# A second layer by seven quarter products, in two phases, in a fused attention and two-layer kernel

## The reference

```python
# q, k, v: 2 x 8 heads x 768 x 64; window 128 and 4 sink keys
a = softmax(where(is_sink | in_window, q @ k.T / 8, -1e9)); x = (a @ v)      # 1536 tokens x 512
h = x @ w_in                                  # layer one, 512 -> 1024
solu = h * softmax(h); ln = (solu - mean) / sqrt(var + 1e-6) * g_ln
x2 = ln @ w_out                               # 1024 -> 512
h2 = x2 @ w2_in                               # layer two, 512 -> 2048
return (maximum(h2, 0) ** 2) @ w2_out         # 2048 -> 512
```

## Time and profile before

| | us |
|---|---|
| timed runs: median (lowest to highest, 3 runs) | 484.2 (483.32 to 484.57) |
| the profiled execution: span | 481.6 |
| TensorE busy | 471.1 |
| VectorE, ScalarE, GpSimd busy | 278.1, 212.9, 103.8 |

### The profile page before, as it was taken

The page is one execution under the profiler, slowest core; times in us unless marked ns, Lnnn a source line. Parts: engine busy times, 40 slices in busy tenths (PEclk is TensorE's granted clock), DMA queues, the critical chain, the costliest instruction groups (busy, mean ns, idle before and its releaser), DMA issues.

```text
span 481.6 us, 7337 instructions
## 1 busy us (share of the span) xinstructions
PE 471.1 (98%) x2634; PEld 382.5 (79%) x2634; DVE 278.1 (58%) x514; ACT 212.9 (44%) x559; POOL 103.8 (22%) x155
## 2 busy tenths in 40 slices
PE   7889999999999999999999999999999999999997
PEld 5667787887788888878888888888888888888885
DVE  3899889898989888767755354322222233222232
ACT  3677777656777666242324253222222232222221
POOL 2366323231321232739930000000000000000000
PEclk9999999999999999999999999999999999999999
DMA  7931437765569424498400000200000020000002
GB/s 214 315 92 50 136 85 215 205 192 159 149 180 219 113 57 120 119 252 240 90 1 0 1 0 1 87 0 0 0 0 0 0 87 1 0 0 1 0 1 87
DMA packets 51990, 41.80 MB, mean 87 GB/s; under 512 B 28088, under 2 KB 38072, under 8 KB 51448
## 3 DMA queue, kind: packets, MB, share of 16 engines
q1 hardware_dynamic: 51192, 40.74, 29.9%
q10 hardware_dynamic: 768, 0.66, 0.5%
HBM read 30.38 MB, written 11.01 MB: 86 GB/s over the span
## 4 chain that ended last, share of the span: by engine, by line
PE 91%; DVE 3%; POOL 2%; ACT 1%; DMA 1%; issue 1%; ACTq 0%; DVEq 0%; POOLq 0%
PE score_ps L1675 27%; PE h_ps L1689 14%; PE w_ps L1516 13%; PE h_ps L1476 12%; PE w_ps L1689 7%; PE wt_ps L1689 7%; PE o_ps L1438 4%; PE score_ps L1404 2%; PE wt_ps L1404 2%; PE wt_ps L1415 1%; DMA x2T<-qT 1%; PE o_ps L1459 1%; POOL pT_own L576 1%; PE w_ps L1541 1%; DVE prob L1095 1%
## 5 line engine op out<-in xcount | busy, mean ns | idle before, releaser
L1675 PE MATMUL score_ps<-x2T_hi,w2in_hi 128*128 (+1 forms) x192 | 74.8, 389 | 0.0
L1675 PE MATMUL score_ps<-x2T_hi,w2in_lo 128*128 (+1 forms) x192 | 74.7, 389 | 0.0
L1675 PE MATMUL score_ps<-x2T_lo,w2in_hi 128*128 (+1 forms) x192 | 74.7, 389 | 0.0
L1328 DVE TENSOR_TENSOR e<-e 128x512 f32<-128x512 f32 x24 | 17.9, 744 | 82.0 <-ACT e L968 82.0
L1328 DVE TENSOR_TENSOR sq<-relu 128x512 f32<-128x512 f32 x24 | 17.2, 717 | 77.0 <-ACT relu L968 77.0
L968 ACT ACTIVATE relu<-score_ps 128x512 f32<-128x512 f32 x24 | 14.3, 597 | 90.5 <-PE score_ps L1675 90.5
L968 ACT ACTIVATE e<-score_ps 128x512 f32<-128x512 f32 x24 | 14.4, 599 | 89.7 <-PE score_ps L1675 89.7
L1675 PEld LDWEIGHTS score_ps<-x2T_lo,w2in_hi 128*128 128x128 f32 x192 | 36.0, 188 | 7.5
L1675 PEld LDWEIGHTS score_ps<-x2T_hi,w2in_hi 128*128 128x128 f32 x192 | 36.1, 188 | 7.5
L1675 PEld LDWEIGHTS score_ps<-x2T_hi,w2in_lo 128*128 128x128 f32 x192 | 36.0, 188 | 7.4
L742 ACT ACTIVATE prob<-sm,nbias 128x132 f32<-128x132 f32 (+1 forms) x96 | 37.6, 393 | 4.1 <-DVE nbias L1019 3.4
(11 more groups left out here) (192 smaller groups left out, 1095.0 us busy)
## 6 DMA issues: line engine op xcount, KB each, us to landing
u_dram<-uT SPq DMA_DIRECT2D x18, 256.0 KB, 3.2
...
w2in<-w_in SPq DMA_DIRECT2D x4, 1024.0 KB, 5.3
...
V<-v SPq DMA_DIRECT2D x12, 256.0 KB, 3.2
x2T<-x_dram SPq DMA_DIRECT2D x12, 256.0 KB, 4.8
x_dram<-x SPq DMA_DIRECT2D x44, 64.0 KB, 2.2
...
```

Of the source, the lines that this page charges most:

```text
L1328: nc.vector.tensor_tensor(sq[f % 2], relu[f % 2], relu[f % 2], ALU.mult).then_inc(sq_ready, 1)
L1675: done = mm(h2_ps[f % 2], ws[:, c, fs], xs[:, c, bass.ts(blk, BLK)], start=(c == 0 and i == 0), stop=(c == MC - 1 and i == 2))
```

## The change

Layer two is done in two phases, and its activation g (16 chunks by all 1536 tokens) is kept whole in SBUF.

Phase one makes g. The tokens are two passes of 768, each in two halves of 384 columns; the hidden chunks are eight pairs j = (chunk j, chunk j + 8). For pairs 0 and 1 each of four quarters (one chunk, one half) is a plain product: 12 matmuls of 384 columns (`quarter`). For pairs 2 to 7 the 2 x 2 block product (two chunks by two halves, the contraction of 512 in two halves of 256) is computed from seven products of sums of quarters instead of eight (`multiply`: 2 passes x 2 contraction chunks x 3 matmuls, 384 columns each). The sums of weights are made by GpSimd per pair (`sum_w2`: four operations of 256 elements; `split_w2`: 512, 512, 512 and 256 elements), the sums of activations once per pass (`sum_x`, `split_x` on VectorE, `round_x` on ScalarE, 768 elements each), and the results are put together in g by ScalarE (copies `copy_p1`, `corner`) and VectorE (five additions of 768 elements, then `gate_row`: relu times itself on 1536). Weights of w2_in are loaded pair by pair.

Phase two multiplies g with w2_out, token tile by token tile: 48 matmuls of 512 columns per tile, g split per tile (`round_g`, `split_g`). w2_out is loaded in eight pieces of two chunks (`wy`) through two raw buffers; the first two tiles go in turns of 4, 4 and 8 chunks. The places of most of these tensors are those of tensors of before that are dead by then.

In layer one, project(9) is cut after 8 of its 24 matmuls, the rest stands behind hidden(11); project(10) writes another PSUM bank than project(11) and the transposes (`x2_bank`), so that `transpose_ln(11)` waits for one square_x2 less; last tile's squares have a place of their own. The loops (`Fori`) of block_b are gone: all is straight-line.

The core of the diff; the removed functions of layer two are those described above, and the small functions left out (`sum_x`, `split_x`, `round_x`, `sum_w2`, `split_w2`, the five additions, `copy_y`) wait for what they read and do one operation each, as told above:

```diff
 QUADS = P // SQ
 MOVES = 16 * QUADS
-NB = T // BLK
-TB = BLK // P
-X2T_AT = (7, 11)
+PASSES = 2
+TS = T // PASSES
+TH = TS // 2
+QH3 = TH // P
+NJ = C2 // 2
+CLASSIC = 2
+QUARTERS = ((0, 0), (1, 0), (1, 1), (0, 1))
+BLOCKS = tuple((j, s) for s in range(PASSES) for j in range(CLASSIC))
+A11, A12, S3, A22, S1, S2, S4 = range(7)
+B11, T2, B21, T3, T1, T4, B22, B12 = range(8)
+PRODUCTS = ((A11, B11, 0, True), (S2, T2, 1, True), (A12, B21, 0, False), (S3, T3, 1, False),
+            (S1, T1, 0, True), (A22, T4, 1, False), (S4, B22, 0, False))
+NP = len(PRODUCTS)
+P_FIRST, P_SECOND, P_CORNER, P_THIRD, P_LOWER, P_LEFT, P_RIGHT = range(NP)
+EARLY_TILES = 2
 LN_EPS, SM_EPS = 1e-6, 1e-9
 
...
+quarter_ps = [score_ps[:, 0:TH], score_ps[:, BANK:BANK + TH]]
+prod_pairs = [(score_pair, wt_pair), (h_pair, wo_pair)]
+y_ps = [score_ps[:, 0:BANK], score_ps[:, BANK:2 * BANK], w0_ps, tr_ps,
+        h_ps[:, 0:BANK], h_ps[:, BANK:2 * BANK], w1_ps, o_ps]
...
+    def load_w2(j):
+        if since(j, 2):
+            sp.wait_ge(w2_split, w2_parts_before(j - 1))
+        for r in range(2):
+            cols = slice((r * NJ + j) * P, (r * NJ + j + 1) * P)
+            sp.dma_start(w2_raw[j % 2][:, :, r, :], w2_in[:, cols].rearrange("(c p) f -> p c f", p=P)
+                         ).then_inc(w2_loaded[j % 2], 16)
+    def load_wy(j):
+        sp.wait_ge(*((wy_split, j - 1) if j >= 2 else (w2_split, w2_parts_before(NJ - 1 + j))))
+        sp.dma_start(wy_raw[j % 2][:, :, :],
+                     w2_out.rearrange("(r j p) m -> p r j m", r=2, p=P)[:, :, j, :]
+                     ).then_inc(wy_loaded[j % 2], 16)
...
+    load_x2T(1, TPB, TPB + QH3, x2T_loaded[1])
     store_x2(NT - 3)
-    load_x2T(1)
-    sp.wait_ge(h_done, 2 * NT)
-    for c in range(C2 // 2):
-        sp.dma_start(w2out[:, 2 * c:2 * c + 2, :],
-                     w2_out[2 * c * P:(2 * c + 2) * P, :].rearrange("(c p) m -> p c m", p=P)
-                     ).then_inc(w2out_loaded[c], 16)
+    sp.wait_ge(lnT_split, len(LN_PARTS) * (NT - 1))
+    load_w2(1)
+    load_w2(2)
     store_x2(NT - 2)
+    load_x2T(1, TPB + QH3, NT - 1, x2T_loaded[2])
     store_x2(NT - 1)
-    load_x2T(2)
-    with sp.Fori(0, NB - 1) as blk:
-        for i in range(TB):
-
-            sp.wait_ge((y_copied_act, y_copied_dve)[i % 2], TB // 2 * blk + (i // 2 + 1))
-            sp.dma_start(out[bass.ds(blk * BLK + i * P, P), :], y[i]).then_inc(y_stored, 16)
-    for i in range(TB):
-        cols = slice(0, DM // 2 if i == TB - 1 else DM)
-        sp.wait_ge((y_copied_act, y_copied_dve)[i % 2], TB // 2 * (NB - 1) + i // 2 + 1)
-        sp.dma_start(out[(NB - 1) * BLK + i * P:(NB - 1) * BLK + (i + 1) * P, cols], y[i][:, cols]
-                     ).then_inc(y_stored, 16)
-    sp.wait_ge(y_stored, 16 * (TB * NB + 1))
+    load_x2T(1, NT - 1, NT, x2T_end_loaded)
+    for j in range(3, NJ):
+        load_w2(j)
+    for j in range(NJ):
+        load_wy(j)
...
+    split_w2(0)
+    inverse_std(NT - 1)
+    split_w2(1)
+    for j in range(CLASSIC, NJ):
+        sum_w2(j)
+        split_w2(j)
...
+    def drain(n):
+        j, s = BLOCKS[n // len(QUARTERS)]
+        r, h = QUARTERS[n % len(QUARTERS)]
+        act.wait_ge(multiplied, n + 1)
+        nc.scalar.copy(g[:, j, r, s * TS + h * TH:s * TS + (h + 1) * TH], quarter_ps[n % 2]).then_inc(corner_ready, 1)
+    def copy_p1(j):
+        act.wait_ge(multiplied, multiplied_before(j) + P_FIRST + 1)
+        nc.scalar.copy(corner_of(j, 1, 0), pair_of(j, 0)).then_inc(p1_copied, 1)
+    def corner(j):
+        act.wait_ge(multiplied, multiplied_before(j) + P_CORNER + 1)
+        nc.scalar.copy(corner_of(j, 0, 0), pair_of(j, 0)).then_inc(corner_ready, 1)
+    def round_wy(j):
+        act.wait_ge(wy_loaded[j % 2], 16 * (j // 2 + 1))
+        act.wait_ge(multiplied, multiplied_before(NJ - 1) + (P_CORNER + 1, P_THIRD + 1, NP)[min(j, 2)])
+        nc.scalar.activation(wy[j][:, :, 0, :], wy_raw[j % 2][:, :, :], ACT.Copy).then_inc(wy_rounded, 1)
+    def round_g(t, part):
+        chunks = g_parts(t)[part]
+        act.wait_ge(g_ready, gates_before(NJ - 1 if len(g_parts(t)) > 1 and part == 0 else NJ))
+        if t < 2:
+            act.wait_ge(multiplied, multiplied_before(NJ - 1) + (P_CORNER + 1, P_LEFT + 1)[t])
+        else:
+            act.wait_ge(y_done, t - 1)
+        nc.scalar.activation(g_hi[t % 2][:, chunks, :], g_tile(t, chunks), ACT.Copy).then_inc(g_rounded, 1)
...
+    round_x(0, B11)
+    round_x(0, B21)
+    round_w2(0)
     hidden_exp(NT - 1)
     hidden_sum(NT - 1)
+    round_x(0, B12)
     for part in range(len(LN_PARTS)):
         round_lnT(NT - 2, part)
+    drain(0)
+    round_x(0, B22)
     for part in range(len(LN_PARTS)):
         round_lnT(NT - 1, part)
+    drain(1)
+    round_w2(1)
+    round_x(0, T1)
+    round_x(0, T2)
+    round_x(0, T3)
+    act.wait_ge(x2_done, NT)
+    round_x(1, B11)
+    round_x(1, B21)
+    for n in range(2, 7):
+        drain(n)
+    round_x(1, B12)
+    round_x(1, B22)
+    drain(7)
+    round_x(0, T4)
+    drain(8)
+    drain(9)
+    act.wait_ge(t_summed[0], 4)
+    round_x(1, T1)
+    round_x(1, T2)
+    drain(10)
+    round_x(1, T3)
+    drain(11)
+    round_w2(2)
+    for n in range(12, 16):
+        drain(n)
+    round_x(1, T4)
+    for j in range(CLASSIC, NJ):
+        copy_p1(j)
+        corner(j)
+        if j + 1 < NJ:
+            round_w2(j + 1)
+    round_g(0, 0)
+    round_wy(0)
+    round_wy(1)
+    round_g(1, 0)
+    round_wy(2)
+    round_wy(3)
+    round_g(0, 1)
+    round_g(1, 1)
+    for j in range(4, NJ):
+        round_wy(j)
...
+    def split_wy(j):
+        dve.wait_ge(wy_rounded, j + 1)
+        nc.vector.tensor_tensor(wy[j][:, :, 1, :], wy_raw[j % 2][:, :, :], wy[j][:, :, 0, :].bitcast(F32),
+                                ALU.subtract).then_inc(wy_split, 1)
...
+    split_x(0, B11)
+    split_x(0, B21)
     square_x2(NT - 3)
     hidden_max(NT - 1, 0)
     hidden_max(NT - 1, 1)
     stats(NT - 1, 0)
     stats(NT - 1, 1)
     aggregate(NT - 1)
+    split_x(0, B12)
     normalize_hidden(NT - 1)
+    split_x(0, B22)
     square_x2(NT - 2)
     for part in range(len(LN_PARTS)):
         split_lnT(NT - 1, part)
+    sum_x(0, T1)
+    sum_x(0, T2)
+    sum_x(0, T3)
     square_x2(NT - 1)
+    split_x(1, B11)
+    split_x(1, B21)
+    split_x(0, T2)
+    split_x(0, T3)
+    split_x(0, T1)
+    sum_x(0, T4)
+    gate_block(0)
+    split_x(1, B12)
+    split_x(1, B22)
+    split_x(0, T4)
+    sum_x(1, T1)
+    sum_x(1, T2)
+    sum_x(1, T3)
+    split_x(1, T2)
+    split_x(1, T3)
+    split_x(1, T1)
+    sum_x(1, T4)
+    gate_block(1)
+    gate_block(2)
+    split_x(1, T4)
+    for j in range(CLASSIC, NJ):
+        sum_2(j)
+        sum_3(j)
+        if j == CLASSIC:
+            gate_block(3)
+        lower_right(j)
+        if j == NJ - 1:
+            split_g(0, 0)
+            split_wy(0)
+        lower_left(j)
+        gate_row(j, 1)
+        if j == NJ - 1:
+            split_wy(1)
+        upper_right(j)
+        if j == NJ - 1:
+            split_g(1, 0)
+            split_wy(2)
+        gate_row(j, 0)
+    split_wy(3)
+    split_g(0, 1)
+    split_g(1, 1)
+    for j in range(4, NJ):
+        split_wy(j)
+    for t in range(NT):
+        if t + 2 < NT:
+            split_g(t + 2, 0)
+        if t % 2:
+            copy_y(t)
...
-        project(n - 2, 0, 24)
+        project(n - 2, 0, 8)
         pe.wait_ge(u_ready, 2 * n)
         hidden(n, 0, 24)
+        project(n - 2, 8, 24)
...
+    def quarter(n):
+        j, s = BLOCKS[n // len(QUARTERS)]
+        r, h = QUARTERS[n % len(QUARTERS)]
+        xs = ((B11, B21), (B12, B22))[h]
+        pe.wait_ge(w2_split, 2 * j + r + 1)
+        pe.wait_ge(xc_split[s][xs[0]], 1)
+        pe.wait_ge(xc_split[s][xs[1]], 1)
+        if n >= 2:
+            pe.wait_ge(corner_ready, n - 1)
+        for c in range(MC):
+            half, cc = c // 2, c % 2
+            for k in range(3):
+                ws, x = ((w2_hi, x_hi), (w2_hi, x_lo), (w2_lo, x_hi))[k]
+                done = mm(quarter_ps[n % 2], ws[j % 2][:, 2 * r + half, cc, :], x(s, xs[half])[:, cc, :],
+                          start=(c == 0 and k == 0), stop=(c == MC - 1 and k == 2))
+        done.then_inc(multiplied, 1)
+    def multiply(j, n):
+        wk, xk, bank, opens = PRODUCTS[n]
+        done = j - CLASSIC
+        pe.wait_ge(w2_split, w2_parts_before(j) + (1, 2, 1, 3, 2, 3, 4)[n])
+        if n == P_FIRST:
+            if j == CLASSIC:
+                pe.wait_ge(corner_ready, corners_before(CLASSIC))
+            elif j == CLASSIC + 1:
                 pe.wait_ge(x2_squared, NT)
+            else:
+                pe.wait_ge(added, 5 * (done - 1))
+        elif n == P_CORNER:
+            pe.wait_ge(p1_copied, done + 1)
+        elif n == P_THIRD:
+            pe.wait_ge(added, 5 * done + 1)
+        elif n == P_LOWER:
+            pe.wait_ge(corner_ready, corners_before(j + 1))
+        elif n == P_LEFT:
+            pe.wait_ge(added, 5 * done + 2)
+        elif n == P_RIGHT:
```

(43 more changed lines are left out.)

424 lines of the change are left out of this document (224 added, 200 removed).

## The result

The changed kernel takes 491.06 us (4 runs, 490.68 to 491.57), the kernel before 483.97 in the same comparison: ratio 1.0149, 95% interval 1.0135 to 1.0164, so 7.1 us slower. The forecast was 3.1 us slower. The profiled execution has a span of 488.9 us, 7.3 above before's 481.6.

What follows compares the result with a forecast made beforehand. TensorE, busy 98% of the span, was taken to bound the kernel. Terms -9.9 - 0.5 + 0.4 + 4.0 + 0.3 + 0.8 + 8.0 = +3.1 on 484.2 gave 487.3 us; 8-in-10 range 481.0 to 491.5.

Steps and rivals of the forecast that it cites:

- project(10), +4.0: Last projections of layer one: TensorE waits ahead of project(10) for a delayed lnT_lo; +4.0 us, bounds 3 to 5.
- rival 3: The clock falls in the waits, at two places, 2.1 us each; +7.3 in total, 491.5 us; chance 0.15.
- The output half is the same 576 matmuls of 512 columns: 0: Layer two's product with w2_out: same matmuls as before at the same pace, so no change.
- Columns, -9.9: Layer two's hidden half: 696 matmuls of 384 columns at 173.3 ns replace 576 of 512; -9.9 us.
- hidden(11), +0.4: Last hidden projection, now behind 8 matmuls of project(9), waits for xT_lo; +0.4 us, 1.6 if normalisations stay slow.
- Transposes, -0.5: Tile 11's transposes no longer wait for square_x2, as the banks differ; -0.5 us.
- drain(2), +0.3: Plain quarters: ScalarE's copy stands behind two roundings needing tile 10 back from DRAM, delaying quarter(4); +0.3 us, 0 to 1.5.
- First product, +0.8: Pair 2's first product uses both banks of the quarters and waits for the last copy; +0.8 us, called certain.
- Products, 0: Pairs 2 to 7: VectorE's and GpSimd's work fits behind the matmuls; 0, to +3 if five pairs lose 0.6 each.
- The turn, +8.0: From last product to output half: waits for VectorE's queue and weights through two raw buffers; +8.0 us, bounds 5.1 to 11.5.

Runs made afterwards that it cites:

- e2: Changed kernel with square_x2(9) moved behind tile 11's maxima and gates on VectorE and the rounding of B12 behind tile 10's on ScalarE; 484.83 us.
- e3: Changed kernel with 21 extra matmuls of 384 columns between quarter(0) and project(10), filling TensorE's wait; 488.15 us.
- e12: Changed kernel with the low places in memory (output weights 0 to 3, eleven activation pieces, w2_sum) moved by 192 bytes; 489.51 us.
- e4: Changed kernel with output weights 4 to 7 loaded from ScalarE's queue straight into their places at the end of the last product; 488.69 us.
- e5: Changed kernel with VectorE's order in the turn changed and the loads left as they are; 488.30 us.
- e10: Changed kernel with VectorE's turn reordered and output weights 2 to 7 loaded in place by SyncE, in order of need, after the last product; 484.81 us.

## Why the prediction was right in its places and wrong in its size

The mechanism was right, fewer columns against new waits, and the waits stand where the forecast put them. What failed were two terms of the sum, which stand first here.

- **What failed: project(10), +4.0, with the clock left out of it.** The wait itself is right: project(10) starts at 211.52, forecast 211.25, by square_x2(9) and the rounding of B12 as named (3.86 us, and e2 takes it away with these two). But the forecast counted the wait alone and kept the clock's fall for rival 3, with a chance of 0.15, at 2.1 us in each of two places. It came in one place, behind the 3.7 us, and cost 1.64 us; e3 gets 1.5 of it back. The term measures 5.5. In the turn the clock stayed up in this trace, after a longest wait of 2.1 us. That rival 3's total (+7.3) is near the measured +7.1 is luck.
- **What failed too: "The output half is the same 576 matmuls of 512 columns: 0".** It measures 1.2 us in tiles 2 to 11 (109.77 us for 108.57 in e12, first to last start), and the same cause adds 0.34 in the products. The trace of before couldn't show it: all its matmuls of layer two run at one pace. The new places stood in the diff.
- **Columns, -9.9: right.** Quarters come at 173.6 and products at 174.05 ns for 173.3; with aligned operands (e12) the products at 173.3. The fixed 13.3 ns hold at 384 columns. The Trainium skill gives N/2.4 + 2.5 ns ("TensorE: Matmul & The Clock Gate", section "Wait — 56ns, not 53.3ns?"), from which 162.5 ns is an estimate; the measurement disagrees.
- **hidden(11), +0.4: right**, 0.5 from start to start. **Transposes, -0.5**: about -0.3; before's wait there (0.29) is gone. **drain(2), +0.3**: nothing.
- **First product, +0.8: right**, 0.79, and by the copy of the last quarter, as forecast.
- **Products, 0: 0.65 too low.** `gate_block(3)` stands ahead of `lower_right(2)` in VectorE's queue, which costs 0.5 in pair 2; slower first starts behind the gaps are the rest.
- **The turn, +8.0: right**, 8.6. The first two waits are VectorE's queue and the last three the raw buffers, as said (e4, e5, e10); a load took 3.6 us, forecast 3.5.
- The forecast's working says that the longest wait of before, behind the start, is 0.85 us. It is 0.93 (at 75.9); nothing else rests on that.

The balance of the missing 4.2: 1.65 for the clock, 1.55 for the places, 0.65 in pair 2, 0.6 in the turn, 0.25 because project(9) already starts that much later than in before, 0.2 in the small terms of the last projections; off come the 0.3 of drain(2) and 0.3 at the end (3.43 us behind the last matmul's start for 3.76). That makes 4.3.
